# Attention and two expert layers on one core: unnormalised split probabilities, division at the x tiles, unrolled program

## The reference

```
def _attn_ref(q, k, v, tau):
    scores = scale * q @ k.T
    thresh = np.max(scores, axis=-1, keepdims=True) - tau
    scores = np.where(scores >= thresh, scores, -1000000000.0)
    scores = scores - np.max(scores, axis=-1, keepdims=True)
    attn = np.exp(scores)
    attn = attn / (np.sum(attn, axis=-1, keepdims=True) + 1e-09)
    return attn @ v

x = attn_out.transpose(0, 2, 1, 3).reshape(2304, 512)
h = x @ w_in;  g = h * np.clip(h + 3, 0, 6) / 6;         x = g @ w_out   # 512 -> 2048 -> 512
h = x @ w2_in; g = h * (1 / (1 + np.exp(-1.702 * h)));   x = g @ w2_out  # 512 -> 2048 -> 512
```

## Time and profile before

| | us |
|---|---|
| median of 3 runs (lowest, highest) | 1228.98 (1228.42, 1233.22) |
| span of the profiled execution | 1225.6 |
| PE busy | 1184.3 (97%) |
| PE weight loads busy | 1020.1 (83%) |
| DVE, ACT, POOL busy | 525.8, 563.2, 545.1 |

### The profile page before, as it was taken

The page is one execution under the profiler, slowest core; times in us unless marked ns, Lnnn a source line. Parts: engine busy times, 40 slices in busy tenths (PEclk is TensorE's granted clock), DMA queues, the critical chain, the costliest instruction groups (busy, mean ns, idle before and its releaser), DMA issues.

```text
span 1225.6 us, 19677 instructions
## 1 busy us (share of the span) xinstructions
PE 1184.3 (97%) x6408; PEld 1020.1 (83%) x6408; DVE 525.8 (43%) x1344; ACT 563.2 (46%) x1002; POOL 545.1 (44%) x457
## 2 busy tenths in 40 slices
PE   5999999989998999989999999999999999999998
PEld 3666677757776677789999999999999999999997
DVE  5777765576656766332222222222222322222221
ACT  5888765566645765444323333233333222222221
POOL 5888655456645565345333333224444222222222
PEclk9999999999999999999999999999999999999999
DMA  4333322141222312323233322112222112222210
GB/s 121 93 103 111 85 58 60 30 118 49 58 58 68 94 35 58 88 68 120 86 113 111 111 102 81 42 57 72 86 86 86 52 52 78 78 77 77 77 52 26
DMA packets 69736, 94.29 MB, mean 77 GB/s; under 512 B 24368, under 2 KB 45872, under 8 KB 69680
## 3 DMA queue, kind: packets, MB, share of 16 engines
q1 hardware_dynamic: 69680, 93.62, 24.8%
HBM read 70.01 MB, written 23.59 MB: 76 GB/s over the span
## 4 chain that ended last, share of the span: by engine, by line
PE 86%; DVE 4%; ACT 4%; issue 4%; POOL 0%; DMA 0%; DVEq 0%; ACTq 0%; SPq 0%; POOLq 0%
PE mm L417 19%; PE score L429 16%; PE tr L417 14%; PE score L427 12%; PE mm L403 10%; PE score L381 5%; PE tr L389 5%; PE mm L427 5%; ACT expd L663 2%; DVE neg_max L537 2%; DVE prob L551 1%; ACT w_hi L684 1%; ACT gate L702 1%; DVE act_f L580 1%; ACT x_hi L698 0%
## 5 line engine op out<-in xcount | busy, mean ns | idle before, releaser
L814 POOL TENSOR_TENSOR g_lo<-act_f,g_hi 128x384 fp32r<-128x384 f32 x192 | 193.8, 1014 | 442.8 <-ACT g_hi L710 442.8
L803 POOL TENSOR_TENSOR prob<-prob,inv_total 128x576 f32<-128x576 f32 x160 | 183.3, 1148 | 179.5 <-DVE inv_total L565 179.1
L403 PE MATMUL mm<-pt,v_raw 128*64 128x320 f32 (+1 forms) x640 | 182.4, 416 | 4.3 <-ACT o_t L678 4.3
L669 ACT ACTIVATE pt<-tr 128x640 f32<-128x640 f32 x160 | 112.3, 702 | 101.1 <-PE tr L389 100.1
L417 PE MATMUL mm<-x_hi,w_hi 128*128 128x384 f32 x432 | 149.6, 346 | 5.7 <-DVE x_lo L572 3.1
L551 DVE SCALAR_TENSOR_TENSOR prob<-score,thresh,expd 128x576 f32<-128x576 f32 x160 | 130.2, 813 | 50.4 <-ACT expd L663 43.7
L663 ACT ACTIVATE expd<-score,neg_max 128x576 f32<-128x576 f32 x161 | 118.9, 739 | 57.4 <-DVE neg_max L537 56.2
L417 PE MATMUL mm<-x_hi,w_lo 128*128 128x384 f32 x432 | 144.8, 335 | 0.0
L417 PE MATMUL mm<-x_lo,w_hi 128*128 128x384 f32 x432 | 144.7, 335 | 0.0
L537 DVE TENSOR_REDUCE neg_max<-score 128x1 f32<-128x576 f32 x161 | 121.5, 755 | 38.8 <-PE score L381 38.5
L403 PEld LDWEIGHTS mm<-pt,v_raw 128*64 128x64 f32 x640 | 77.1, 136 | 68.1 <-issue 22.0
(11 more groups left out here) (64 smaller groups left out, 2266.8 us busy)
## 6 DMA issues: line engine op xcount, KB each, us to landing
x_raw<-x_t_scratch SPq DMA_DIRECT2D x24, 768.0 KB, 5.8
q_raw<-in_qT SPq DMA_DIRECT2D x68, 144.0 KB, 2.8
k_raw<-in_kT SPq DMA_DIRECT2D x68, 144.0 KB, 2.9
stage<-in_w_in SPq DMA_DIRECT2D x16, 512.0 KB, 6.4
stage<-in_w_out SPq DMA_DIRECT2D x16, 512.0 KB, 6.5
x_t_scratch<-o_t SPq DMA_DIRECT2D x32, 144.0 KB, 2.4
part_t_scratch<-y_out SPq DMA_DIRECT2D x6, 768.0 KB, 4.2
part<-part_t_scratch SPq DMA_DIRECT2D x6, 768.0 KB, 7.8
```

The source lines that it names most:

```text
L403: m = pe.matmul(pv_out[0:HD, 0:n_q], v_raw[:, par, c, :], pt[:, c, cols], start=c == 0, stop=c == QB - 1)
L669: act.activation(pt[:, :, j * P:j * P + P], turned_p.rearrange("p (c n) -> p c n", c=QB), ACT.Copy).then_inc(pt_copied, 1)
L803: pool.tensor_tensor(p, p, inv_total[:, s % RING:s % RING + 1].broadcast_to([P, S]), ALU.mult).then_inc(norm_done, 1)
L814: pool.tensor_tensor(g_lo[:, c, :], act_f[:, c % 2, :], g_hi[:, c, :], ALU.subtract).then_inc(g_lo_done, 1)
```

## The change

It rewrites the attention and the order of all five programs. What each part does:

- **Slots.** The last 64 rows of the two heads of a pair share one block of 128 rows, so a pair has 9 slots; that slot's scores take 8 matmuls instead of 4. The fully unrolled program has 144 attention slots and 12 more, g = 0 to 155.
- **Probabilities** are not normalised. ACT writes the exponential straight into `prob`, DVE masks it there, and `normalize` is gone. `turn` waits for the mask alone. ACT copies the transposed block as `pt_hi` and DVE writes the rest as `pt_lo`, both float32r; `turn` of block x+1 waits for `pt_lo` of x.
- **Product with V.** V is split into high and low side by side (128 columns, on ACT and POOL), and `prob_v` is 10 float32r matmuls per group, 40 per pair, 128 output rows; the halves are stored apart in `o_parts`.
- **Division.** One inversion per pair on DVE; the inverses go to DRAM in elements of 4 bytes and come back spread over the partitions. POOL makes each x tile of the first step: `x_raw + x_low`, times `inv_b` (`make_x`), and SP stores it for the second step.
- **Tiles of the first step** are 288 tokens wide, 8 of them. Six are mixed into the slots (before: three of six tiles of 384). A mixed **piece** is 12 matmuls in one slot: a whole `h` chunk, or half of a `y` block. Pieces begin at slot 46; every ninth slot (every seventh in the last batch) has none. 87 of the 96 pieces lie in the slots 46 to 143.
- **Thresholds** move from DVE to POOL. Maxima run one block further ahead: DVE does `row_max(g+2)`, then `mask(g+1)`.
- **Order in a slot.** PE: scores(g+2), the mixed piece of slot g, turn(g-2), products with V. ACT: gate of the piece of slot g-1, `high_turned(g-2)`, exponential(g+2), copy of a product with V, `high_g` of the piece of slot g-1, q, k and v.

```diff
+    NARROW, TT = HALF, 384
+    MIXED = 2 * (B - 1)
+    for b in range(1, B):
+        g0, every = BATCH_SLOTS * b + SLOTS + 1, 8 if b + 1 < B else 6
+        for p in range(2 * PIECES):
+            PIECE[g0 + p + p // every] = (2 * (b - 1) + p // PIECES, p % PIECES)
...
@@ PE
+            def turn(x):
+                pe.wait_ge(mask_done, x + 1)
+                wait(pe, pt_lo_done, x)
+                for c in range(CHUNKS):
+                    m = pe.transpose(turned_p[:, c * P:c * P + P], prob[:, x % PROBS, c * P:c * P + P], ident[:, :])
+                m.then_inc(turned, 1)
+            def prob_v(n):
+                k, side = n % 4, (n % 4) // 2
+                width = GROUP_COLS[k][1]
+                pe.wait_ge(pt_lo_done, group_last(n) + 1)
+                pe.wait_ge(v_lo_done, 2 * (n // 4) + side + 1)
+                wait(pe, o_copied, n)
+                for low, p_part in enumerate((pt_hi, pt_lo)):
+                    for c in range(CHUNKS):
+                        m = pe.matmul(pv_out[:, 0:width], v_hl[:, side, c, :], p_part[:, GROUP_BUF[k], c, 0:width],
+                                      start=low == 0 and c == 0, stop=low == 1 and c == CHUNKS - 1)
+                m.then_inc(pv_done, 1)
+            def mixed_piece(ti, p):
+                if p < FC:
...
+                    wait(pe, mix_drained, mix_item(ti, p))
+                    h_chunk(mix_out, p, w_hi[0], w_lo[0], width).then_inc(mix_filled, 1)
+                    return
+                m, second = divmod(p - FC, 2)
+                if not second:
+                    pe.wait_ge(mix_drained, mix_item(ti, p))
...
+            for g in range(END):
+                if g + 2 < G:
+                    scores(g + 2)
+                if g in PIECE:
+                    mixed_piece(*PIECE[g])
+                if 0 <= g - 2 < G:
+                    turn(g - 2)
+                n = at_slot(PV, g)
+                if n is not None:
+                    prob_v(n)
@@ DVE
+            for g in range(END):
+                done = PIECE.get(g - 1)
+                if done is not None:
...
+                        gated(ti, mix_out, p).then_inc(mix_drained, 1)
...
+                        drain_y(ti, mix_out, (p - FC) // 2).then_inc(mix_drained, 1)
+                if g + 2 < G:
+                    row_max(g + 2)
+                if g + 1 < G:
+                    mask(g + 1)
+                if 0 <= g - 2 < G:
+                    low_turned(g - 2)
+                if kind(g) == SLOTS - 1 and g < G:
+                    invert(g // SLOTS)
+                if g in SPLIT_X:
+                    low_x(*SPLIT_X[g])
@@ ACT
+            for g in range(END):
+                i, s = divmod(g, SLOTS)
+                done = PIECE.get(g - 1)
+                if done is not None and done[1] < FC:
+                    act.wait_ge(mix_filled, mix_item(*done) + 1)
+                    gates(done[0], mix_out, done[1])
+                if 0 <= g - 2 < G:
+                    high_turned(g - 2)
+                if g + 2 < G:
+                    exponent(g + 2)
+                n = at_slot(O_COPY, g)
+                if n is not None:
+                    copy_o(n)
+                if done is not None and done[1] < FC:
+                    act.wait_ge(mix_drained, mix_item(*done) + 1)
+                    high_g(*done)
...
@@ POOL
+            def make_x(ti, k):
...
+                pool.tensor_tensor(place, place, x_low[:, k, 0:width], ALU.add).then_inc(x_added, 1)
+                pool.wait_ge(x_added, KC * ti + k + 1)
+                pool.tensor_tensor(place, place, inv_b[:, k, :], ALU.mult).then_inc(x_made, 1)
```

More of the change, by code:

```diff
@@ L584, in drain_y, with mask @@
-            def drain_y(step, bank, m, tile):
+            def mask(g):
+                r = g % RING
+                dve.wait_ge(exp_done, g + 1)
+                dve.wait_ge(thresh_done, g + 1)
+                p = prob[:, g % PROBS, 0:S].rearrange("p (a n) -> p a n", a=2)
+                dve.scalar_tensor_tensor(out=p, in0=score[:, g % 2, :, 0:HALF], scalar=thresh[:, r:r + 1], in1=p,
+                                         op0=ALU.is_ge, op1=ALU.mult, accum_out=total[:, g // SLOTS % 2, kind(g):kind(g) + 1]
+                                         ).then_inc(mask_done, 1)
@@ L591, in drain_y @@
                 if partial is None:
-                    return dve.tensor_scalar(y_part(y_out, step, m), bank, scale, None, ALU.mult)
-                return dve.scalar_tensor_tensor(out=y_part(y_out, step, m), in0=bank, scalar=scale,
-                                                in1=y_part(part, step, m), op0=ALU.mult, op1=ALU.add)
-            def pair(i, unit, mlp):
-                for s in range(SLOTS):
-                    g = SLOTS * i + s
-                    mask(g, s)
-                    row_max(g + 1, s + 1)
-                    threshold(g + 1, s + 1)
-                    sum_total(g, s)
-                    if mlp is not None:
-                        mlp(s)
-                    invert(g, s)
@@ L621, in _ @@
-            attention(dve, pair, mix)
-            for k in range(KC):
-                low_x(MIXED, k)
-            def tile_body(step, tile, units):
-                base = first_item(step, tile)
+                    return dve.tensor_scalar(y_part(y_out, ti, m), bank, scale, None, ALU.mult)
+                return dve.scalar_tensor_tensor(out=y_part(y_out, ti, m), in0=bank, scalar=scale,
+                                                in1=y_part(part, ti, m), op0=ALU.mult, op1=ALU.add)
+            row_max(0)
@@ L627, in tile_body @@
+            for ti in range(MIXED, len(TILES)):
+                base = first_item(ti)
                 for c in range(FC):
-                    gated(step, h_bank[c % len(h_bank)], c, tile).then_inc(mm_drained, 1)
-                if not is_last(tile):
+                    gated(ti, h_bank[c % len(h_bank)], c).then_inc(mm_drained, 1)
+                if ti + 1 < len(TILES):
                     for k in range(KC):
-                        low_x(tile + 1, k)
-                for m in range(blocks_y(step)):
-                    wait(dve, mm_filled, base + FC + m + 1)
-                    drain_y(step, y_bank[m], m, tile).then_inc(mm_drained, 1)
@@ L636, in _ @@
[L636 to L637 removed]
+                        low_x(ti + 1, k)
+                for m in range(blocks_y(ti)):
+                    dve.wait_ge(mm_filled, base + FC + m + 1)
+                    drain_y(ti, y_bank[m], m).then_inc(mm_drained, 1)
         @block.scalar
         def _(act):
[L644 to L648 removed]
@@ L695, in high_x, with q_place, heads_free @@
-            def high_x(tile, k):
-                if k == 0:
-                    wait(act, x_loaded, 16 * (tile + 1))
-                act.activation(x_hi[:, k, :], x_raw[:, k, :], ACT.Copy).then_inc(x_hi_done, 1)
-            def gates(step, bank, c):
+            def q_place(h):
+                first = (h % 2) * (S + TAIL)
+                return q_sp[:, first:first + S]
+            def heads_free(h):
+                if h > 1:
+                    act.wait_ge(scores_ready, SLOTS * (h // 2 - 1) + (SLOTS if h % 2 else MID + 1))
@@ L782, in _ @@
+                high_g(ti, FC - 1)
+                if ti + 1 < len(TILES):
+                    for k in range(KC):
+                        high_x(ti + 1, k)
+                for n in range(2):
+                    if ti == MIXED:
+                        high_half_unit(1, 2, n)
+                    if step > 0 and t < UNITS and step + 1 < STEPS:
+                        high_half_unit(step + 1, t, n)
         @block.gpsimd
@@ L835, in mix @@
[L835 to L848 removed]
+            low_q(0)
```

980 lines of the change are left out of this document (497 added, 483 removed).

## The result

| | before | after |
|---|---|---|
| median of four runs of each (lowest, highest of after) | 1230.74 us | 1443.0 us (1440.77, 1445.52) |
| ratio | | 1.172 (95%: 1.169 to 1.175) |
| span of the profiled execution | 1225.6 us | 1441.4 us |

A forecast was written before the change was run, and what follows sets the result against it. PE outright bounds only the final tiles; in mixed slots a chain over PE, ACT and DVE decides. Span 14.5 + 129 + 460 + 28 + 58 + 599 = 1288.5 us, with 3.4 more 1292 us, 5% slower; range 1215 to 1345.

The forecast's parts named there:

- the tail: Behind slot 143: nine left pieces, 28 us, and two tiles of the first step, 58 us.
- a granted clock of 1.00: Sign expected in the profile after: PE's granted clock stays at 1.00, as in every stretch before.
- rival 4: PE's clock falls to 1.2 GHz as PE idles 2 us and more per h slot: about 1440 us; chance 0.05.
- its loads wait for the 4-byte store: Slots 0 to 45, first x tile: POOL's make_x work and loads behind the store, 5 us added.
- rival 3: Loads of x tiles come late and hold POOL; 10 us for each of three batches, 1322 us; chance 0.12.
- A: Time of slots 0 to 45, without mixed pieces: forecast 129 us, bounds 113 and 145.
- 3.3: waits for nobody: Mixed slots, second half of a y block: no wait, 3.3 us each, 20 of them, 66 us.
- B: Time of mixed slots 46 to 143: forecast 460 us, 4.7 a slot, bounds 307 and 505.
- 10% more: Upper bound of the mixed slots' term: 505 us against the forecast 460.
- masks that wait for thresholds: Sign that the forecast is wrong: masks in the attention slots waiting for POOL's thresholds; no size given.
- Rivals 1 and 2: Mixed slots: 1, PE's work decides, 1140 us, chance 0.08; 2, the chain is shorter, 1253 us, chance 0.08.
- turning point: Mixed-stretch time at which the change would turn from slower to faster: 399 us, 4.07 a slot.

The follow-up runs named there:

- experiment 1: The changed kernel with the turn and the products with V ahead of the mixed piece on PE: 1282.6 us, ratio 1.046.
- experiment 5: The changed kernel with extra matmuls of 192 columns, results unused, ahead of mixed h pieces alone: 1416.1 us, ratio 1.152.
- experiment 3: The changed kernel with inverses stored in runs of 36 bytes instead of 4 (x tiles divided by other rows' sums): 1391.9 us, ratio 1.132.
- 7: The changed kernel with turn and products with V ahead of the piece, thresholds first on POOL, inverses in 36-byte runs: 1235.0 us, ratio 1.004.
- 12: The changed kernel with turn first, inverses transposed on PE (512-byte runs), later weight splitting, threshold ahead only of the fourth q's low part: 1235.9 us, ratio 1.005.
- experiment 16: As 12, with inverses transposed two slots later, behind the piece, except for the last pair of each batch: 1216.8 us, ratio 0.989.
- experiment 10: The changed kernel, piece still ahead of the turn, with inverses transposed on PE (512-byte runs), thresholds first, weights after h chunks: 1372.4 us, ratio 1.115.
- experiment 9: As experiment 1, with the last weights split behind the last h chunk and the last x tile stored a load later: 1285.0 us, ratio 1.045.
- experiment 6: The changed kernel with the threshold issued first in POOL's slot, ahead of the low parts of q, k and v: 1429.6 us, ratio 1.161.
- experiment 2: The changed kernel with a piece's gate, gating and low part one slot earlier, the gate ahead of pt_hi; PE's order kept: 1313.1 us, ratio 1.068.

## Why the prediction was wrong

The step that failed is the sum, not the chain: the forecast took the granted clock at 1.00, put the store of the inverses at next to nothing, and priced slots and tail without slack. Of the 153 us over its span, the store holds 51 and the clock in the mixed slots about 20. Some 80 are left, 21 in slots 0 to 45, 30 in the mixed slots and 30 in the tail; for them there are readings of the timelines, and no experiment that takes them away.

**Right: direction and mechanism.** The order on PE and on ACT decides. PE waits for DVE's gating 38 times for 73.6 us, 1.9 each (forecast: about 45 waits of 2 to 3 us), the gate stands behind `pt_hi` and the exponential, and either order that lifts it out gives 130 to 160 us. The forecast priced the mixed stretch at 460 us against 307 of PE's own work, so 153 for the order; experiment 1 took 143 us from this stretch.

**Right: the small prices.** Products with V were taken at 0.1325 us, the low end of their bounds. Timeline of PE in experiment 1, a group of 256 columns at full clock, five matmuls in a row:

```profile
304.10 0.84 PE L453 MATMUL mm<-pt_hi,v_hl 128*128 128x256 f32 x5
304.79 0.40 PE L453 MATMUL mm<-pt_lo,v_hl 128*128 128x256 f32 x2
```

0.69 us for five, or 0.138 each. `low_turned` takes 0.82 us (forecast 0.83), gating 0.46 (0.455), gate 0.51 (0.50). The 18 tiles and the start were met within 2 us.

**Wrong: "a granted clock of 1.00".** This step failed outright. I had rival 4 at 0.05 because every stretch of before shows 1.00. But PE was busy for 94% or more of each of those stretches, so its rows can't speak for a kernel that idles 2 us per slot. The clock was 0.81, 0.86 and 0.85 in the three stretches. The Trainium skill, TensorE: Matmul & The Clock Gate, section Why this matters for your kernels, warns of idle gaps between bursts of matmuls, but of longer ones. The trace agrees with the warning and goes beyond it: gaps of 1.94 us as above, coming back slot after slot, were enough. Still rival 4 isn't what happened, though its 1440 us lies within 3 us of the result: it asked 150 us of the clock, and experiment 5 shows about 20 in the mixed slots. That the number was met is luck: the other terms below were short too. The lower clock lengthens PE's part of a slot, and in the timeline above the scores at least lie beside work of ACT.

**Mis-sized: the 4-byte store.** It had "its loads wait for the 4-byte store" inside a term of 5 us and 10 us for each of three batches in rival 3. It costs 51 us (experiment 3). Rival 3 was right in kind where it looked, at the x tiles: 20 us against its 30. As much again, 24 us, lies where nothing in the prediction looked, behind the loads of weights. By stretches, 38 us are in slots 0 to 45, of the 59 us that this term was short, 8 in the mixed slots and 5 in the tail.

**Mis-sized: slots 0 to 45 otherwise.** With the store mended, A is 144 to 152 us (experiments 3, 7 and 12) against 129. The forecast spread bunches of q, k and v evenly at 0.2 us a slot. In experiment 16 these slots run from 2.4 to 4.3 us, two of 5.4 and 5.8 excepted, and about half of them are over 2.9. I read that as work on q, k and v (1.4 us on POOL, 0.7 on ACT) that lands on the loop at once; no experiment took it away.

**Mis-sized: the mixed slots.** Beside the clock, the `y` halves: the 20 second halves were "3.3: waits for nobody" and took a mean of 4.79 us, the 15 first halves behind a piece 5.46 against 4.45. With store and thresholds mended (experiment 10) they are still 4.30 and 4.98, and `h` behind `h` is 6.16 against 5.7: B is 506 there against 460. A sum of links without any slack is near a lower bound, and my "10% more" for the upper bound (505) was just what experiment 10 needed, with a granted clock of 0.89 there.

**Mis-sized: the tail.** 121 us against 86. On the chain that ends last stand two waits for loads of weights, 9.3 and 6.5 us, which the forecast didn't have, and a load of `inv_b` of 7.8 us; the last weights stand on POOL ahead of `g_lo`; and the granted clock is 0.85. Experiment 9 took 11 us from it, which the stretches ahead of it lost; in experiment 16 it is 98.

**Missed: thresholds.** The forecast named "masks that wait for thresholds" only as a sign of being wrong. They cost 2 to 13 us (experiment 6).

**Rivals 1 and 2** fell. Their turning point, 399 us for the mixed stretch, held only for a kernel whose other parts come out as forecast: experiment 1 has 375 there and is slower than before, since slots 0 to 45 and the tail are 74 us over; experiment 16, with 358 there and 29 us over elsewhere, is faster.

## What to carry to other kernels

When an instruction that others wait for (here the gate) stands in its queue behind one that waits for the same producer's next work (here the copy of the turn), the two engines take turns instead of overlapping; look for this in the order of the two queues before counting the work saved. Once PE idles in each slot, take its clock from no trace in which it was busy: bound the term at both levels, and then ask how much of PE's part lies on the chain. A store in elements of 4 bytes is to be priced by its number of elements and by every load that shares the DMA engines for that time, whichever queue issues it; a transpose on PE that makes long runs of it (0.37 us in its record) costs little, provided it doesn't stand in front of something that PE could do meanwhile.

## What the runs showed of the hardware

- 1152 elements of 4 bytes, with the loads issued behind them, kept the DMA engines busy for some 13 us at 18 to 26 GB/s; loads of 512 KB issued behind them landed after 15.0, 14.8 and 15.4 us. With the store on a second queue it was 13.8, and with runs of 36 bytes 4.9.
- The granted clock fell again and again in slots in which PE idled for about 2 us, and it could fall inside the burst that came behind the gap. In the timeline of after above it is low from the first matmuls behind the gap on; in experiment 2, behind a gap of 2.29 us, it falls later:

```profile
304.70 0.40 PE L433 MATMUL score<-k_hi,q_sp 128*128 128x288 f32 x1 [2.29 <-DVE prob L560]
304.94 0.29 PE L433 MATMUL score<-k_lo,q_sp 128*128 128x288 f32 x1
...
305.74 0.29 PE L470 MATMUL mm<-g_hi,w_hi 128*128 128x288 f32 x1
305.87 0.38 PE L470 MATMUL mm<-g_lo,w_hi 128*128 128x288 f32 x1
306.05 0.44 PE L470 MATMUL mm<-g_hi,w_lo 128*128 128x288 f32 x1
306.29 0.44 PE L470 MATMUL mm<-g_hi,w_hi 128*128 128x288 f32 x1
```

Distances go from 0.13 us (2.4 GHz) to 0.24 (1.2 GHz) at 306.05.
